# An attention kernel fused with an MLP: where the product with V stands inside a slot

## The reference, cut to what matters

```python
# q, k, v: 4 batches x 8 heads x 576 x 64; U 576x32, V 32x576, w_ch1 512x2048, w_ch2 2048x512
q_rot, k_rot = rotate(q), rotate(k)
scores = scale * np.matmul(q_rot, k_rot.transpose(0, 1, 3, 2))
attn = np.exp(scores - max); attn = attn / (sum + 1e-09)
x = np.matmul(attn, v) -> (B, S, H*D)             # per batch 576 x 512
h = x.transpose(0, 2, 1) @ U @ V                   # mixing along the sequence, rank 32
u = x + h.transpose(0, 2, 1)
out = u + np.maximum(u @ w_ch1, 0) @ w_ch2
```

## Time and profile before

| | |
|---|---|
| median of three runs | 781.98 us (781.86, 781.98, 785.59) |
| the profiled execution | 785.53 us; span of its instructions 783.7 us |
| PE busy | 719.9 us (92%), 4252 matmuls |
| ACT, POOL, DVE busy | 448.2, 455.3, 405.0 us |
| SyncE's DMAs | 116.98 MB, 50.1% of the 16 engines' span |
| chain that ended last | PE 75%, DVE 9%, ACT 6%, issue 4%, DMA 3%, POOL 2% |
| mean granted TensorE clock | 0.98 |

### The profile page before, as it was taken

How to read it: one execution, slowest core, us unless ns; L and a number is a source line. 1 busy time by engine, 2 the same in 40 slices (tenths; PEclk the granted TensorE clock), 3 DMA queues, 4 the chain that set the end, 5 groups by cost and what they waited for, 6 DMA issues and landing times.

```text
span 783.7 us, 12244 instructions
## 1 busy us (share of the span) xinstructions
PE 719.9 (92%) x4252; PEld 645.1 (82%) x4252; DVE 405.0 (52%) x669; ACT 448.2 (57%) x959; POOL 455.3 (58%) x349
## 2 busy tenths in 40 slices
PE   0888888799999999999999999999999699999998
PEld 0777776689999787989899988889999579899896
DVE  2687887665555776444454456565554642112111
ACT  1787886567576766555565565666665333333332
POOL 2565667348576775485584876647533226556553
PEclk9999998699999999999999999999999999999999
DMA  7966566453656635727547265282622135345342
GB/s 236 238 163 164 144 165 196 105 164 100 203 143 211 148 118 160 230 81 208 177 136 238 91 187 169 95 235 72 175 90 96 41 128 167 134 156 171 126 162 80
DMA packets 74700, 119.59 MB, mean 153 GB/s; under 512 B 27152, under 2 KB 27280, under 8 KB 72848
## 3 DMA queue, kind: packets, MB, share of 16 engines
q1 hardware_dynamic: 73600, 116.98, 50.1%
q10 hardware_dynamic: 1040, 1.84, 0.8%
HBM read 81.04 MB, written 9.44 MB: 115 GB/s over the span
## 4 chain that ended last, share of the span: by engine, by line
PE 75%; DVE 9%; ACT 6%; issue 4%; DMA 3%; POOL 2%; ACTq 0%; POOLq 0%; DVEq 0%; SPq 0%
PE ps L927 23%; PE ps L945 22%; PE ps L855 9%; PE ps L842 8%; PE ps L875 7%; DVE negmax L705 2%; ACT prob L569 2%; PE ps L868 1%; DVE ptl L713 1%; DVE pth L717 1%; PE ps L909 1%; ACT pth L579 1%; DMA sin_t<-in_sin 1%; DMA stack<-raw 1%; PE ps L897 1%
## 5 line engine op out<-in xcount | busy, mean ns | idle before, releaser
L495 POOL TENSOR_TENSOR w1l<-w1u,w1h 128x512 fp32r<-128x512 f32 x96 | 124.0, 1292 | 245.1 <-ACT w1h L610 245.1
L705 DVE TENSOR_REDUCE negmax<-ps 128x1 f32<-128x576 f32 (+1 forms) x160 | 120.3, 752 | 82.5 <-PE ps L842 80.2
L579 ACT ACTIVATE pth<-ps 128x512 fp32r<-128x512 f32 (+1 forms) x192 | 107.7, 566 | 90.0 <-PE ps L875 88.0
L788 DVE SCALAR_TENSOR_TENSOR htl<-ps,hth 128x384 fp32r<-128x384 f32 x96 | 53.5, 557 | 186.1 <-ACT hth L621 185.9
L842 PE MATMUL ps<-stack 128*128 128x288 f32 (+1 forms) x640 | 119.6, 310 | 22.9 <-DMA stack<-raw 21.5
L569 ACT ACTIVATE prob<-ps,negmax 128x576 f32<-128x576 f32 (+1 forms) x160 | 118.0, 738 | 38.6 <-DVE negmax L705 38.2
L927 PE MATMUL ps<-uth,w1h 128*128 128x384 f32 x384 | 132.8, 346 | 0.7 <-DVE utl L779 0.5
L927 PE MATMUL ps<-uth,w1l 128*128 128x384 f32 x384 | 129.9, 338 | 0.0
L927 PE MATMUL ps<-utl,w1h 128*128 128x384 f32 x384 | 129.7, 338 | 0.0
L621 ACT ACTIVATE hth<-ps 128x384 fp32r<-128x384 f32 x96 | 47.2, 491 | 139.9 <-PE ps L927 139.7
L501 POOL TENSOR_TENSOR w2l<-w2u,w2h 128x512 fp32r<-128x512 f32 x96 | 123.7, 1289 | 4.5 <-ACT w2h L614 4.5
(11 more groups left out here) (60 smaller groups left out, 1074.8 us busy)
## 6 DMA issues: line engine op xcount, KB each, us to landing
w1u<-in_w SPq DMA_DIRECT2D x96, 256.0 KB, 2.7
w2u<-in_w SPq DMA_DIRECT2D x96, 256.0 KB, 2.7
stack<-raw SPq DMA_DIRECT2D x64, 288.0 KB, 4.2
raw<-in_qk SPq DMA_DIRECT2D x14, 1152.0 KB, 5.4
stack<-raw SPq DMA_DIRECT2D x60, 144.0 KB, 3.9
v2u<-in_v SPq DMA_DIRECT2D x16, 320.0 KB, 3.8
res<-scratch_u SPq DMA_DIRECT2D x18, 256.0 KB, 3.5
out<-res SPq DMA_DIRECT2D x18, 256.0 KB, 2.2
```

Source lines behind the costliest of these rows:

```text
L495: nc.gpsimd.tensor_tensor(w1l[:, at], w1u[:, at], w1h[:, at], ALU.subtract).then_inc(w1_lo, 1)
L579: nc.scalar.activation(pth[rows, keys, queries], source, ACT.Copy).then_inc(pt_hi, 1)
L705: nc.vector.tensor_reduce(negmax[0:WT[t], t:t + 1], scores_of(n, WT[t]), AX.XY, ALU.max, negate=True).then_inc(maxed, 1)
L788: nc.vector.scalar_tensor_tensor(htl[:, i % 2], up_bank(), 0.0, hth[:, i % 2], ALU.max, ALU.subtract).then_inc(relu_lo, 1)
```

## The change

`sequence(n)` now holds the product with V too. It pairs the slot's MLP parts with the other items, of which the product with V is the first. So in a slot with MLP parts the product with V stands behind the first part; in a slot without parts it stands where it stood. Where a slot has mix items as well, these shift by one place against the MLP parts. TensorE, ScalarE and VectorE follow the new order; GpSimd takes the new order of its mix and MLP items. Plan, banks and waits are as before.

```diff
 def sequence(n):
 
-    parts, mixes = MLP_AT.get(n, []), mixes_of(n)
+    parts = [("mlp", *x) for x in MLP_AT.get(n, [])]
+    others = [("pv", *x) for x in pv_of(n)] + [("mix", *x) for x in mixes_of(n)]
     out = []
-    for i in range(max(len(parts), len(mixes))):
-        out += [("mlp", *x) for x in parts[i:i + 1]] + [("mix", *x) for x in mixes[i:i + 1]]
+    for i in range(max(len(parts), len(others))):
+        out += parts[i:i + 1] + others[i:i + 1]
     return out
...
-                        elif x[1] == "natural" and x[0] < B - 1:
+                        elif of == "mix" and x[1] == "natural" and x[0] < B - 1:
                             split_x(x[0], x[2])
...
-                if n >= MERGED:
-                    for half in pv_of(n):
-                        lower_half(*half)
...
                     for of, *x in sequence(n):
                         if of == "mlp":
                             mlp(*x)
+                        elif of == "pv":
+                            lower_half(*x)
                         else:
                             mix(*x)
...
-                    for half in pv_of(n):
-                        add_halves(*half)
                     for of, *x in sequence(n):
                         if of == "mlp":
                             mlp(*x)
+                        elif of == "pv":
+                            add_halves(*x)
                         else:
                             mix(*x)
...
-                    for half in pv_of(n):
-                        times_v(*half)
                     for of, *x in sequence(n):
                         if of == "mlp":
                             mlp(*x)
+                        elif of == "pv":
+                            times_v(*x)
                         else:
                             mix(*x)
```

## The result

The changed kernel took 793.18 us (median of 4 runs, 791.05 to 794.73) against 783.79 us for the kernel before: ratio 1.0116, interval 1.0082 to 1.0149. Measured twice more beside the experiments, it took 789.2 us against 784.56 (1.0062, 1.0030 to 1.0094) and 790.52 us against 785.09 (1.0078, 1.0052 to 1.0104). So the change is slower beyond doubt, by 4.6 to 9.4 us. The forecast was +3.4 us, 785.3 us, with 787.6 us as the upper end: the sign and the main mechanism hold, the size is too small, and all three results lie outside the range, the first one farthest.

What follows compares the result with a forecast made beforehand. The prediction took TensorE as the bound; its terms 0, -1.05, +2.8, +0.85 and +0.8 sum to +3.4 us, on the median 781.98 giving 785.3 us. The forecast's own range was 783.6 to 786.8, the 8-in-10 range 780.5 to 787.6.

Steps and rivals of the forecast that it cites:

- term C: Slots 127 and 128: natural 4 moves behind up(43,1) on GpSimd, so low 4 waits for xl 4; +2.8 us.
- slots 62, 137 and 152: Same shape as slot 77, weights there: Relu and roundings run 1.28 us earlier, paying for the copy behind them; 0.
- term B: Waits at the product in slots 132 and 135 that an MLP part now covers; -1.05 us (0 to -1.8).
- term E: Slot 77: the product's copy stands behind Relu, w1h and w2h on ScalarE, delaying slot 79's scores; +0.8 us.
- The bound: TensorE, busy 418.46 of 426.00 us from 174 to 600 us; reordering can win at most part of 7.5 us.
- A: 19 slots with the LAST unit: the wait behind five 64-row turns stays whoever is next; 0, at best -1.9 us.
- rival 3: Faster: the 0.1 us behind LAST goes in 19 slots, slot 128's hole halves; -2.3 us, 779.7 us; chance 0.1.
- rival 1: The granted clock falls behind slot 128's hole, adding 1.7 us to the forecast: 787.0 us; chance 0.25.
- D: Slot 87, low 3 waits for the product's bank, +0.55 us; slots 90 to 92 likewise, +0.3; together +0.85 us.
- Rival 2: The order is neutral, as POOL, ACT and DVE have more slack: -0.25 us, 781.7 us; chance 0.2.

Runs made afterwards that it cites:

- bothback: The changed kernel, but mix items keep their old pairing and the product stays in front where the first part is up(i,1); 784.51 us, ratio 1.0000.
- mixpair: The changed kernel, product still behind the first part, but mix items keep their old pairing with the MLP parts; 784.5 us, ratio 1.0005.
- only127: The kernel before, with the changed order in slot 127 alone; 788.81 us, ratio 1.0043.
- copyfirst: The changed kernel, but ScalarE copies the product's lower half directly behind Relu, ahead of both roundings, where the first part is up(i,1); 788.64 us, ratio 1.0041.
- up1stay: The changed kernel, but the product stays directly behind the turns in the 12 slots whose first part is up(i,1); 788.61 us, ratio 1.0049.
- after_third: The changed kernel measured a third time, unchanged; 790.52 us, ratio 1.0078.

## Why the prediction was wrong, point by point

The step that failed is the sum: it put at nothing three things that then cost time. These are the fall of the granted clock behind the hole of term C (1.5 us in six of eight executions, but not in the one profiled with the first result), slots 62, 137 and 152 (0.9 us), and the place where term B's gain in slot 132 is paid back (0.5 us in slot 134). The first result has on top a wait in slot 107 that the sum did not hold either (3.2 us with the clock behind it), and term E at 1.7 us instead of 0.8.

- **The bound** held: all of the change is in TensorE's holes and in the clock behind two of them, and what moving the product can win is small (0.4 us in bothback).
- **A** held at 0. Behind five turns of 64 rows the next matmul starts 0.45 us later in the changed kernel too, where it is an MLP part:

```profile
521.82 0.52 PE L875 MATMUL ps<-ident,prob 64*128 64x64 f32 x5
522.27 0.44 PE L927 MATMUL ps<-uth,w1h 128*128 128x384 f32 x1
```

  That is the 0.45 us of the earlier trace rows, with another successor. So it is not the product's own wait, and rival 3 falls.
- **B**, -1.05 us, came out at -0.4. Slot 132 gives -0.6 us (forecast -0.75), and slots 135 and 136 together -0.3 us, as forecast. What failed is what the sum left out: in slot 132 the new pairing also puts turned_u 1 behind up(47,0), its utl comes later, and the turns of slot 134 wait for it, which costs 0.5 us:

```profile
518.09 0.60 PE L868 MATMUL ps<-ident,prob 128*64 128x128 f32 x4 [0.43 <-DVE utl L779]
```

  In mixpair and bothback, which keep the old pairing of the mix items, slot 134 costs nothing more than before.
- **C**, the hole of slot 128, held in place, cause and nearly in size: +2.8 forecast, +2.5 measured in two executions, 0.4 us of them at the turns, where the prediction had none. What failed is to leave the clock behind it to a rival with a quarter of the chances: of eight executions of kernels with this hole, six have the fall (15.2 to 15.3 us), two do not (13.7 to 13.8). So this step costs 4.0 us more often than not, and rival 1's 1.7 us (1.5 measured) belonged in the likeliest case. only127 shows it alone. Even so rival 1's 787.0 us is too low, for the other reasons.
- **D**, +0.85 us, measured +0.71, by two errors that offset each other: slots 87 to 89 cost 0.3 us instead of 0.55 (slot 87 loses 0.7 and slot 88 takes 0.4 back), slots 90 to 92 cost 0.4 instead of 0.3. The mechanism held: low 3 in slot 87 waits for the addition, which answers to the earlier trace rows:

```profile
277.54 0.60 PE L887 MATMUL ps<-ident,xt 128*64 128x128 f32 x4
278.68 0.50 PE L897 MATMUL ps<-xh,us 128*128 128x512 f32 x1 [0.55 <-DVE xt L727]
```

- **E** held in its mechanism (copyfirst shows it), but 0.8 us with 1.35 as the upper end was too low for some executions: 0.7, 1.0 and 1.7 us in the three of the changed kernel. The upper end let the copy stand behind w1h and w2h from w1h's old start; in the first execution the load held w1h back for another 0.45 us, and the row maximum came 1.84 us after that of the earlier trace rows.
- "In slots 62, 137 and 152 ... just pays for the copy behind them: 0" failed: each shows about 0.3 us, 0.9 us over 62-77 and 137-159. up1stay, with the product back in these slots, loses them all, and copyfirst, with the copy ahead of the roundings, loses most.
- **Not in the sum at all: slot 107.** It has the order of slot 77 and a load that is later still. It made 3.2 us of the first execution and 0 and 1.0 us of the others. Leaving it out was a gap, for nothing in the prediction says why; but the table behind after_third gives the change no share in it, and in the first result it is bad luck as far as the runs show.
- Rival 2 (neutral) falls with C; bothback shows that it is right, in sum, for moving the product in 27 slots with the mix items left alone.

By the table, stretch by stretch from 62-77 to 137-159, the first execution has 0.3 + 1.7 + 0.7 + 3.2 + 2.5 - 0.4 + 0.6 = 8.6 of its 9.0 us from slot 58 on. The third has 0.3 + 1.0 + 0.7 + 1.0 + 4.0 - 0.45 + 0.6 = 7.2 us, less 1.0 us at the end of the program, which varies by that much between executions; that leaves the 6.3 us of the table within rounding. So slot 107 weighs most in the first, and slot 128 with the clock behind it in the third.

What stays open: why the w1 load of step 29 takes 4.8 to 7.6 us from issue to landing, and whether the earlier issue of the next load has a part in it; why the clock falls behind the hole of slot 128 in some executions only, and what makes up the rest of the first result's distance to the two later ones, as one of its four runs was profiled.

## What to carry to other kernels

When a list of work is re-paired, look at every engine's own list and not at TensorE's alone: here one entry that moved behind two unrelated subtractions on GpSimd cost 3.7 us of the 4.6 to 9.4 (only127). Price a wait by what else stands behind the waiting instruction on its engine, above all a wait for a DMA, and give it the longest landing the trace shows. Before a hole is put down to a change, look for it in executions that have the old order at that place: slot 107 would have passed for 3 us of price. Put the operand that is needed next ahead of the one that is needed later, on each engine that prepares them.

## What the runs showed that was not expected

A hole of 2.5 us (0.4 and 1.9 us, with 1.3 us of work between) on a TensorE that is busy on both sides brought a stretch at the lower clock in six executions of eight, worth another 1.5 us, and the hole of 1.88 us of slot 108 brought one in the first execution, while the holes of up to about 1.5 us in the same stretch of the program brought none. The first 54 slots, whose code is the same in all kernels here, took between 121.5 and 126.7 us in the 14 profiled executions, more than the whole effect of most edits; the lengths of later slots repeat within 0.05 us unless a load or the clock is in them. So a single execution, read slot by slot, tells where the time goes, which ten timed runs do not; what it can't tell is whether a wait for a load will be there the next time.
